# Attention and two gated convolutions on one core: weight halves on another engine, a new order of ScalarE's gate work, other PSUM banks for the outputs, taps loaded earlier

## The reference

```
scores = q @ k.T / 8 - slope[h] * |rel|      # 4 batches, 8 heads, 576 rows, head 64
attn   = softmax(scores where 0 <= rel < 128) @ v        # x: 4 x 576 x 512
h      = relu(x @ w_in)                                  # 512 -> 1024
x2     = (h * sigmoid(conv3(h))) @ w_out                 # 3 taps per column, 1024 -> 512
y      = (sigmoid(conv5_causal(x2)) * (x2 @ w_val)) @ w_out2      # 5 taps, 512 -> 512
```

## Time and profile before

| | |
|---|---|
| median of 3 runs | 499.18 us (497.71 to 499.33) |
| profiled execution | 499.55 us, span 497.8 us |
| PE busy | 451.1 us, 91% |
| VectorE, ScalarE, GpSimd busy | 313.3 (63%), 280.7 (56%), 90.7 us (18%) |
| mean granted PE clock | 0.976 of full |
| chain that ended last | PE 63%, ACT 14%, DVE 12%, issue 6% |
| DMA | 25.80 MB, mean 52 GB/s; 218 GB/s in the first 12 us |

### The profile page before, as it was taken

The page is one execution under the profiler, slowest core; times in us unless marked ns, Lnnn a source line. Parts: engine busy times, 40 slices in busy tenths (PEclk is TensorE's granted clock), DMA queues, the critical chain, the costliest instruction groups (busy, mean ns, idle before and its releaser), DMA issues.

```text
span 497.8 us, 9662 instructions
## 1 busy us (share of the span) xinstructions
PE 451.1 (91%) x3424; PEld 416.8 (84%) x3424; DVE 313.3 (63%) x1120; ACT 280.7 (56%) x788; POOL 90.7 (18%) x132
## 2 busy tenths in 40 slices
PE   3588589979999999998998999997998999999996
PEld 3468568978889998997987988997887989898996
DVE  5396666875782677466774577747676376737741
ACT  2476763486453964386553784378545586358131
POOL 3200999140000310031000130013000040004000
PEclk9999859998999999998999999998999999999999
DMA  8557103010211012101210012111210100010011
GB/s 218 143 160 276 42 1 87 0 32 17 60 44 59 1 43 65 63 10 42 65 44 30 30 24 65 36 53 44 52 44 14 59 1 1 2 49 1 1 49 47
DMA packets 38927, 25.80 MB, mean 52 GB/s; under 512 B 22752, under 2 KB 35040, under 8 KB 38880
## 3 DMA queue, kind: packets, MB, share of 16 engines
q1 hardware_dynamic: 38880, 25.20, 17.7%
HBM read 20.47 MB, written 4.72 MB: 51 GB/s over the span
## 4 chain that ended last, share of the span: by engine, by line
PE 63%; ACT 14%; DVE 12%; issue 6%; SPq 2%; DMA 2%; POOL 1%; DVEq 0%; ACTq 0%
PE bank L782 15%; PE bank L784 14%; PE bank L783 14%; PE bank L763 7%; PE bank L742 7%; PE bank L728 6%; ACT conv L423 4%; DVE conv L600 3%; DVE conv L608 2%; DVE probs L515 2%; DVE gate L656 2%; ACT conv L429 2%; ACT bank L416 2%; DMA taps<-taps 2%; ACT probs L387 1%
## 5 line engine op out<-in xcount | busy, mean ns | idle before, releaser
L782 PE MATMUL bank<-g_hi,w_hi 128*128 128x288 f32 x384 | 120.3, 313 | 6.6 <-DVE neg_max L515 5.0
L782 PE MATMUL bank<-x_hi,w_hi 128*128 128x290 f32 (+1 forms) x384 | 117.6, 306 | 7.2 <-DVE conv L608 5.8
L357 POOL TENSOR_TENSOR g_lo<-conv,g_hi 128x288 fp32r<-128x288 f32 x64 | 51.8, 811 | 355.4 <-ACT g_hi L437 355.4
L783 PE MATMUL bank<-x_lo,w_hi 128*128 128x290 f32 (+1 forms) x384 | 115.0, 299 | 0.0
L784 PE MATMUL bank<-x_hi,w_lo 128*128 128x290 f32 (+1 forms) x384 | 114.6, 298 | 0.0
L784 PE MATMUL bank<-g_hi,w_lo 128*128 128x288 f32 x384 | 113.3, 295 | 0.0
L783 PE MATMUL bank<-g_lo,w_hi 128*128 128x288 f32 x384 | 113.2, 295 | 0.0
L600 DVE SCALAR_TENSOR_TENSOR conv<-bank,taps,conv 128x288 f32<-128x288 f32 (+1 forms) x128 | 65.5, 513 | 62.3 <-ACT conv L423 62.0
L782 PEld LDWEIGHTS bank<-x_hi,w_hi 128*128 128x128 f32 x384 | 73.8, 192 | 10.4 <-DVE conv L608 8.7
L782 PEld LDWEIGHTS bank<-g_hi,w_hi 128*128 128x128 f32 x384 | 72.2, 188 | 8.5 <-DVE neg_max L515 5.9
L387 ACT ACTIVATE probs<-probs,neg_max 128x192 f32<-128x192 f32 (+2 forms) x144 | 62.0, 432 | 29.1 <-DVE neg_max L515 27.8
(11 more groups left out here) (43 smaller groups left out, 539.8 us busy)
## 6 DMA issues: line engine op xcount, KB each, us to landing
w_raw<-panels SPq DMA_DIRECT2D x12, 512.0 KB, 6.6
y_t<-y_sb SPq DMA_DIRECT2D x32, 144.0 KB, 1.8
q_tile<-q_t SPq DMA_DIRECT2D x32, 128.0 KB, 3.0
k_all<-k_t SPq DMA_DIRECT2D x16, 256.0 KB, 3.6
v_tile<-v_tiles SPq DMA_DIRECT2D x16, 256.0 KB, 2.7
q_tile<-q_t SPq DMA_DIRECT2D x8, 64.0 KB, 2.4
k_all<-k_t SPq DMA_DIRECT2D x4, 128.0 KB, 2.6
v_tile<-v_tiles SPq DMA_DIRECT2D x4, 128.0 KB, 3.1
```

Of the source, the lines that this page charges most:

```text
L357: pool.tensor_tensor(g1_lo[:, m, :], conv[n % DEPTH][:, :], g1_hi[:, m, :], ALU.subtract).then_inc(g1_lo_done, 1)
L782: pe.matmul(out, w_hi[:, p, col:col + P], hi(k), start=start, stop=False)
L783: pe.matmul(out, w_hi[:, p, col:col + P], lo(k), start=False, stop=False)
```

## The change

- Taps: SP loads them after tile 1, ahead of panels 1 and 2; ScalarE waits for them in the first `center_rows`.
- Weights: GpSimd only rounds panels 4 to 7 (beats 1, 3, 5, 7 of chunk 0); VectorE subtracts for them, half a panel a step, in steps 12 to 19. GpSimd splits panels 8 and 9 in beats 12 and 16 of chunk 0, 10 and 11 in beats 0 and 4 of chunk 1.
- ScalarE: in a beat, `g1_high` comes after `center_rows` and `gate_rows`; `gate2_rows` moves from the next chunk's up beats to beats 22 and 23 of its own chunk, two a beat, behind `out_rows`.
- Banks: `out` uses banks 0, 1, 4, 5 and waits accordingly.
- Steps of odd chunks run on beats 10 to 21.

```diff
-OUT_BANK = (5, 4, 6, 7)
+OUT_BANK = (0, 1, 4, 5)
...
-            if c % 2 == 1 and c < CHUNKS - 1 and 0 <= j - VAL0 - 1 < FIRST:
-                return STEPS * (c // 2 + 1) + j - VAL0 - 1
+            if c % 2 == 1 and c < CHUNKS - 1 and 0 <= j - DOWN0 + 2 < FIRST:
+                return STEPS * (c // 2 + 1) + j - DOWN0 + 2
...
             load_values(1)
+            sp.dma_start(taps1[:, :, :], taps1_in).then_inc(taps_loaded, 16)
+            sp.dma_start(taps2[:, :, :], taps2_in).then_inc(taps_loaded, 16)
             load_panel(1)
             load_panel(2)
-            sp.dma_start(taps1[:, :, :], taps1_in).then_inc(taps_loaded, 16)
-            sp.dma_start(taps2[:, :, :], taps2_in).then_inc(taps_loaded, 16)
...
# GpSimd
             def slot(step):
-                if FIRST <= step and step % 2 == 0 and step < STEPS:
-                    split_panel(P_OUT + 2 + (step - FIRST) // 2)
+                pass
...
-                if c == 0 and j in (2, 6):
-                    split_panel(P_OUT + (j - 2) // 4)
+                if c == 0 and j < KW and j % 2 == 1:
+                    round_panel(P_OUT + j // 2)
                 if c == 0 and j in (DOWN0, DOWN0 + 4):
-                    split_panel(PANELS - 2 + (j - DOWN0) // 4)
+                    split_panel(P_VAL + (j - DOWN0) // 4)
+                if c == 1 and j in (0, 4):
+                    split_panel(P_OUT2 + j // 4)
...
# ScalarE
             def center_rows(c, m):
                 n, at = KW * c + m, 2 * (c % 2)
                 act.wait_ge(hidden_done, n + 1)
+                if n == 0:
+                    act.wait_ge(taps_loaded, 32)
...
-                if c < CHUNKS and 2 <= j < KW + 2:
-                    g1_high(c, j - 2)
                 if c < CHUNKS and j < KW:
                     center_rows(c, j)
                 if c < CHUNKS and 1 <= j < KW + 1:
                     gate_rows(c, j - 1)
-                if c > 0 and j < KW and j % 2 == 1:
-                    gate2_rows(c - 1, j // 2)
+                if c < CHUNKS and 2 <= j < KW + 2:
+                    g1_high(c, j - 2)
...
                 if c > 0 and j >= OUT0:
                     out_rows(c - 1, j - OUT0)
+                if c < CHUNKS and j >= OUT0 + 2:
+                    gate2_rows(c, 2 * (j - OUT0) - KM)
+                    gate2_rows(c, 2 * (j - OUT0) - KM + 1)
...
-            act.wait_ge(taps_loaded, 32)
             walk(slot, close, beat)
...
# VectorE
-                if step < FIRST and step >= FIRST - 2 * P_OUT:
-                    low_of_w_in(step - FIRST + 2 * P_OUT)
+                if 0 <= step - STEPS + 2 * P_VAL < 2 * P_VAL:
+                    low_of_panel(step - STEPS + 2 * P_VAL)
...
# TensorE: up
-                    if c > 1:
-                        pe.wait_ge(y_kept, KM * (c - 2) + OUT_BANK.index(bank) + 1)
-                elif c > 0:
-                    pe.wait_ge(x2_lo_done, KM * (c - 1) + bank + 1)
-                    pe.wait_ge(conv2_done, KM * (c - 1) + bank + 1)
+                else:
+                    second_input_left(c - 1, bank)
+                if c > 1 and bank in OUT_BANK:
+                    pe.wait_ge(y_kept, KM * (c - 2) + OUT_BANK.index(bank) + 1)
...
# TensorE: out
-                if c + 1 < CHUNKS:
+                if c + 1 == CHUNKS:
+                    pe.wait_ge(y_kept, KM * (c - 1) + m + 1)
+                elif bank < KM:
+                    second_input_left(c + 1, bank)
+                else:
                     attention_left(c + 1, bank)
                     pe.wait_ge(g1_done, KW * (c + 1) + UP_BANK.index(bank) + 1)
-                else:
-                    pe.wait_ge(y_kept, KM * (c - 1) + m + 1)
```

More of the change, by code:

```diff
@@ L135, in attention_and_gated_convolutions @@
         w_rounded = sem("w_rounded")
-        w_in_split = sem("w_in_split")
+        w_halves_split = sem("w_halves_split")
         w_split = sem("w_split")
@@ L563, in kept_early, with low_of_panel @@
                 return step + LOOK if step is not None and last_of_run(step) else None
-            def low_of_w_in(i):
+            def low_of_panel(i):
                 n, at = i // 2, i % 2 * (PANEL // 2)
@@ L570, in low_of_w_in @@
                 dve.tensor_tensor(w_lo[:, n, cols], w_raw[:, n, cols], w_hi[:, n, cols],
-                                  ALU.subtract).then_inc(w_in_split, 1)
+                                  ALU.subtract).then_inc(w_halves_split, 1)
             def slot(step):
@@ L787, in panels_split @@
             def panels_split(through):
-                pe.wait_ge(w_split, (through - P_OUT) * (PANEL // PIECE))
+                if through <= P_VAL:
+                    pe.wait_ge(w_halves_split, 2 * through)
+                else:
+                    pe.wait_ge(w_split, (through - P_VAL) * (PANEL // PIECE))
             def attention_left(c, bank):
@@ L798, in attention_left, with second_input_left @@
                     pe.wait_ge(x_lo_done, end_of_steps(c) // PAIRS)
+            def second_input_left(c, bank):
+                if c >= 0:
+                    pe.wait_ge(x2_lo_done, KM * c + bank + 1)
+                    pe.wait_ge(conv2_done, KM * c + bank + 1)
             def up(c, m):
@@ L806, in up @@
                     if c == 0:
-                        pe.wait_ge(w_in_split, 2 * P_OUT)
+                        panels_split(P_OUT)
                 if bank >= KM:
                     attention_left(c - 1, bank)
-                    if c > 1:
-                        pe.wait_ge(y_kept, KM * (c - 2) + OUT_BANK.index(bank) + 1)
-                elif c > 0:
-                    pe.wait_ge(x2_lo_done, KM * (c - 1) + bank + 1)
-                    pe.wait_ge(conv2_done, KM * (c - 1) + bank + 1)
+                else:
+                    second_input_left(c - 1, bank)
+                if c > 1 and bank in OUT_BANK:
+                    pe.wait_ge(y_kept, KM * (c - 2) + OUT_BANK.index(bank) + 1)
                 product(banks[bank][:, 0:READ], lambda k: (P_IN + k, m * P),
@@ L823, in val @@
                 else:
-                    pe.wait_ge(conv2_done, KM * c + m + 1)
+                    second_input_left(c, m)
+                    if m in OUT_BANK:
+                        pe.wait_ge(y_kept, KM * (c - 1) + OUT_BANK.index(m) + 1)
                 if m == 0:
```

## The result

The changed kernel took **473.13 us** (median of 4 runs, 472.08 to 474.47) against 498.62 for the kernel before on the same chip: ratio 0.949, interval 0.946 to 0.952. A second set of runs of the same code later gave 470.79 (470.04 to 471.68), ratio 0.944, interval 0.940 to 0.948. The forecast was 470.5 with a range of 463 to 479.

A forecast was written before the change was run, and what follows sets the result against it. TensorE (PE), busy 451 of 497.8 us, was taken as the bound, with only its gaps and slow clock to win. 499.55 - 6.0 - 2.1 - 5.8 - 6.0 - 5.0 - 5.0 + 1.0 = 470.65; predicted median 470.5 us, range 463 to 479.

The forecast's parts named there:

- A: Kernel start: taps loaded early end ScalarE's 8.0 us wait, moving everything behind up; -6.0 us, bounds 5 to 7.
- rival 2: Start bound by transfers: tiles 1 and 2 take up the taps' stall, gain shrinks to 3, 473.5 us; chance 0.10.
- B, first half: Chunk 0 gate stage: ScalarE's `g1_high` placed last, so `center` no longer waits for `gated`; last `gated` 2.6 us earlier.
- B, second half: Steps 12 to 19 running alone: low parts on VectorE at 0.93 us each, +0.5 us; both halves together -2.1.
- Rival 1: Steps 12 to 19 bound by VectorE, every low part waiting out a GpSimd subtraction: both halves +2, 475 us; chance 0.15.
- rival 5: Steps 12 to 19 running alone at full clock with their low parts hidden: 467 us; chance 0.07.
- C: First val product: PE's seven waits of 0.83 us for `gated` of row 4 go; -5.8 us, at least 4 of 7.
- the ring: Gate stage before: `g1_hi`, `center`, VectorE's tap, `gated`, next `g1_hi` wait in turn, 1.78 us a beat against PE's 1.60.
- D and E: Odd chunks: D, first attention step a beat later, -6.0 for waits, -5.0 for clock; E, outputs in freed banks, -5.0 us.
- Second gates at the chunk's end: ScalarE's last two beats: table load and gates fit before output 3 is needed, by 0.1 us; cost 0, bounds 0 to 1.3.
- Rivals 3 and 4: Six chunk ends: 3, output 3 late by 1.3 us, 478.5, chance 0.10; 4, PE waits behind load and gates, 506, chance 0.03.
- F: Chunk 1: panel 11's split delays GpSimd's `g1_low` 3, 2.2 us of ScalarE and about 1 of PE; +1.0 us (0 to 2).

## Why the prediction was right, and where it was not

The time lies 2.6 us above the forecast in the first set and 0.3 in the second. The sum as written gives 470.25 on the scale of the median; the forecast says 470.5.

**A, taps: right.** Forecast 6.0, measured 6.1 alone, 6.0 in the repeat, 4.6 in the first profile. No queue took it up, so rival 2 is out. The 1.4 us of difference goes in the main with PE's pace: its attention products ran at half their later speed until about 18.4 us in the first profile (scores of tile 1 1.65 us at 12.20, had 1.48 and later 0.82), and until about 14 us in the repeat. The two do not follow each other strictly (with second gates undone the pace rose at 13.8 us, and the first up product started at 37.25).

**B, first half: right in size, half right in cause.** 2.34 us against 2.6, all of which I gave to ScalarE's order. With the order alone undone the wait is 6.1 instead of 4.9, 1.26 us. With the order kept and the low parts undone it is the whole of the old 7.2: GpSimd's splits of panels 4 and 5 are back among the `g1_low`, and `center_rows` waits 2.5 us for it in chunk 0. So the new order gains nothing there unless GpSimd is relieved too, and the prediction did not name that condition.

**B, second half: the price of one low part was right, the price of the run was not.** I took 0.93 us; the eight took 1.00 in the mean (7 of them 1.09, 1.21, 1.21, 1.22, 0.68, 1.21 and 0.68). But the run grew by 1.3 us against the trace of before, not 0.5. The window view over the run, of the kernel before, of the changed kernel and of the version with the splits behind it (busy us of PE, PEld, DVE, ACT, POOL, then the clock):

```profile
63.99:79.43 15.44, 14.10 (x104) 10.48 (x105) 10.03 (x46) 9.33 (x33) 15.12 (x24) 0.73 0.20 52
```

```profile
57.09:73.83 16.74, 14.25 (x105) 10.42 (x105) 16.17 (x57) 9.36 (x32) 14.44 (x18) 0.73 0.18 49
```

```profile
55.66:68.96 13.30, 12.54 (x104) 9.32 (x104) 11.76 (x57) 9.18 (x32) 0.00 (x0) 0.83 0.22 61
```

Before, VectorE was idle for 5.4 of 15.44 us. Eight low parts of 1.00 us are more than that: VectorE is now busy for 16.2 of 16.74 us and sets the run. The normalisation is not what grew, as its ten full-width instructions take 4.8 us in the run before and after. The failed step is the overlap, the way from 0.93 us a low part to +0.5 for the run, for which no row was given. The step lengths named there (3.0 us against 2.7, 2.1 against 1.4) would give 4 x 0.3 + 4 x 0.7 = 4.0 us if each were paid, so that 0.5 came near 1.3 is partly luck. How much of the 1.3 is the edit's stays open: the old code of this stretch takes 15.60 us with the low parts undone and 16.04 with the taps alone, so against these it is between 0.7 and 1.3.

Rival 1 named this engine and forecast +2 for B; the measured B is -1.0, between it and the forecast. What I did not ask was the other half of the contention: I let GpSimd run into the lone run as if only its end mattered. Without that neighbour the same low parts leave the run at 13.30 us, 2.1 less than before, and at 12.69 with the clock held at full, 2.75 less. I had given 3.5 less as the lower end. So rival 5 named a price that is nearly reached, but only with GpSimd out of the run, which this code does not have.

**C, the val stage: right that it goes, wrong about the size.** The seven waits are gone, 5.8 us. Yet the six chunks without a late panel gained more than forecast. The list of waits shows only the first product's 0.83; the timeline shows three stalls. This is PE's timeline in the val stage of chunk 7, in the kernel with the taps alone, which has the old order:

```profile
448.69 0.40 PE L783 MATMUL bank<-x_hi,w_hi 128*128 128x288 f32 x1 [0.83 <-DVE conv L609]
...
450.48 0.40 PE L783 MATMUL bank<-x_hi,w_hi 128*128 128x288 f32 x1
...
452.26 0.40 PE L783 MATMUL bank<-x_hi,w_hi 128*128 128x288 f32 x1
```

Products follow each other every 1.60 us; here the starts are 1.79 and 1.78 apart. Each product waits by the code for the next row's `gated`, and 1.78 is the pace of the ring in the earlier trace rows; the waits are too brief to be listed. Each start after a stall is a matmul of 0.40 instead of 0.29 us. The up stage lost 13.79 - 12.80 = 0.99 us and the val stage 7.82 - 7.34 = 0.48: 1.47 us a chunk, not 0.83. The row was in my view (the earlier trace rows has the ring at 1.78 us a beat); I used it for chunk 0 alone and did not say that val, at 1.60, would run into it product by product.

**D and E, odd chunks: right in sum, and unevenly so in the parts.** For chunks 3 and 5 the two steps were to bring (2.02 + 1.68 + 1.7) = 5.4 us each; 6.77 less C's 1.47 leaves 5.3. E is its 1.68 us and a little more, 1.94 by the two runs with steps undone. D's cause was ScalarE's lag first (of 2.02 us and the 1.7 of the clock behind it, 3.7 in all, only 0.95 comes back with the step in its old place), the later beat second. The clock gave back its 1.7 us, as the window of the changed kernel at 1.00 shows against the earlier trace rows.

**Second gates at the chunk's end: right.** Rivals 3 and 4 needed a PE wait on `y_sb`; there is none in the list. ScalarE's timeline at the end of chunk 1 goes as laid out, with the gates behind the load at once, as in the earlier trace rows:

```profile
147.42 1.28 ACT L444 ACT_TABLE_LOAD   x1
148.71 0.78 ACT L444 ACTIVATE gate<-gate 128x288 f32<-128x288 f32 x2
149.40 0.38 ACT L462 COPY y_sb<-bank 128x288 f32<-128x288 f32 x1
149.67 0.78 ACT L444 ACTIVATE gate<-gate 128x288 f32<-128x288 f32 x2
150.35 0.40 ACT L417 ACTIVATE bank<-bank 128x290 f32<-128x290 f32 x1
```

Only chunk 1 pays, for the fourth gate of chunk 0, 0.75 us, where I had written "level again by row 2".

**F, panel 11: right mechanism, wrong size.** 2.46 us against 1.0 (I gave 0 to 2 as bounds). The step that failed in size is the one from 2.2 us of ScalarE's delay to 1 us of PE, for which the prediction has no row: PE paid for nearly all of it. ScalarE's delay of 2.50 (its timeline, then GpSimd's, of the changed kernel) reached PE in two places, 1.32 and 1.39:

```profile
103.64 0.50 ACT L426 ACTIVATE conv<-bank,taps 128x288 f32<-128x288 f32 x1 [2.50 <-POOL g_lo L357]
...
99.96 2.82 POOL L351 TENSOR_TENSOR w_lo<-w_raw,w_hi 128x256 fp32r<-128x256 f32 x4
102.73 1.58 POOL L357 TENSOR_TENSOR g_lo<-conv,g_hi 128x288 fp32r<-128x288 f32 x2
```

## What to carry to other kernels

An engine that is moved off a job is not gone: ask where its remaining work now falls, and whether the engine that took the job has to share with it; holding GpSimd back until VectorE was through brought 6.4 to 8.7 us more (464.44 against 470.79 and 473.13). By the profiles 3.5 us of it lie in the shared stretch and 2.5 in chunk 1. Read a wait's price from the starts in the timeline, not from the list: one of 0.83 us stood for 1.47. And when two delays share a margin, undoing either brings little back (here 0.14 and 0.58 us of 1.47 in an even chunk, and the listed wait in neither), so undo both together, which was not done here, before saying what removed a wait. Last, run one unaltered stretch several times before explaining half a microsecond in it: the lone run beside GpSimd took 16.7 to 17.6 us over five kernels with the same code in it.

## What the runs showed of the hardware that was not expected

- VectorE and GpSimd stretch each other in SBUF: a 128x512 subtraction 0.68 to 1.22 us, two 128x192 normalisations 0.55 to 1.57, GpSimd's cast 0.62 to 0.8.
- At the start PE's products take about twice their later time (scores of four matmuls 1.65 against 0.82 us), until 18.4 us in the first profile and 13.9 in the repeat of the same code. The page of the profile prints 9 tenths and the window view 1.00 for this time, but the trace has no clock record there: its first one begins at 18.39 and at 13.89 us, at full clock, just where the products take their later time. So the printed clock at the start is the lack of a record, and the pace is that of the lower level.
- In the lone run the clock is worth little while VectorE sets the pace: 13.30 us with the lower level at its start, 12.69 without.
- A stretch at the lower clock can come when PE has only short waits ahead of it (0.60 over 8 us at 72; in the 8 us before, the longest wait was 0.60 us), in one profile. In both of the changed kernel, with PE busy for 2.9 and 3.4 of the 4 us before 72 against 3.1 here, this stretch stands at full pace. Not explained.
- In some profiles up stages of even chunks ran at 136.1 instead of 133.3 ns a matmul, 0.27 us a stage, at a granted clock of 1.00: all of them in the first profile of the changed kernel and with panels 10 and 11 early, one with the steps undone. Not explained.
